# A delta-rule attention with two expert layers on one core: solves placed earlier, expert blocks six steps behind attention

## What is computed

```
k_n = k / (norm(k) + 1e-6);  state = 0            # 48 x 48 per head
for t in range(768):
    y[t]  = q[t] @ state
    v_old = k_n[t] @ state
    state = state + beta[t] * outer(k_n[t], v[t] - v_old)
```

```
P = exp(x @ w_gate - max);  8 times: rows, then columns of P normalised, P *= N / E
out = sum over e of P[:, e] * (relu(x @ w1[e]) @ w2[e])
```

## Time and profile before

| | us |
|---|---|
| median of 3 runs | 2405.42 (2396.09 to 2406.7) |
| the profiled execution | 2400.81 |
| its span, first to last instruction | 2399.0 |
| TensorE busy | 2252.4 (94%) |
| DVE busy | 1015.1 (42%) |
| ScalarE busy | 611.0 (25%) |
| GpSimd busy | 106.1 (4%) |
| mean granted clock of TensorE | 0.958 |
| a kT load (512 KB), issue to landing, median | 5.2 |

### The profile page before, as it was taken

How to read it: one execution, slowest core, us unless ns; L and a number is a source line. 1 busy time by engine, 2 the same in 40 slices (tenths; PEclk the granted TensorE clock), 3 DMA queues, 4 the chain that set the end, 5 groups by cost and what they waited for, 6 DMA issues and landing times.

```text
span 2399.0 us, 43062 instructions
## 1 busy us (share of the span) xinstructions
PE 2252.4 (94%) x18100; PEld 2089.4 (87%) x18100; DVE 1015.1 (42%) x1831; ACT 611.0 (25%) x1021; POOL 106.1 (4%) x106
## 2 busy tenths in 40 slices
PE   3878988898999999999999999999999996899998
PEld 3878988798999999899899899989999886899998
DVE  6655554426432323333233333333333325566664
ACT  2322222231111111111111111111111122566664
POOL 0000000000000000000000000000000000222221
PEclk7789989899999999999999999999999997899999
DMA  7554344322000000000000000000000012666651
GB/s 246 171 146 120 114 122 115 102 76 100 27 27 1 27 1 27 27 1 27 1 27 27 1 27 1 27 26 2 1 1 1 14 40 79 221 228 209 232 199 61
DMA packets 153378, 173.92 MB, mean 72 GB/s; under 512 B 82124, under 2 KB 113008, under 8 KB 153218
## 3 DMA queue, kind: packets, MB, share of 16 engines
q1 hardware_dynamic: 148354, 159.29, 20.8%
q0 software_dynamic: 4864, 12.20, 1.4%
HBM read 145.50 MB, written 28.71 MB: 73 GB/s over the span
## 4 chain that ended last, share of the span: by engine, by line
PE 88%; DVE 5%; DMA 2%; SPq 2%; issue 2%; ACT 1%; POOL 0%; POOLq 0%; ACTq 0%; DVEq 0%
PE psA L1480 21%; PE psH L1495 15%; PE psB L1480 8%; PE psB L1495 7%; PE psY L1495 7%; PE psY L1589 7%; PE psA L1265 4%; PE psH L1381 4%; PE psA L1576 3%; PE psB L1576 3%; PE psY L1396 3%; PE psB L1364 1%; PE psB L1354 1%; PE psB L1323 1%; DMA r_scratch<-sr 1%
## 5 line engine op out<-in xcount | busy, mean ns | idle before, releaser
L1480 PE MATMUL psA<-X,wh 128*128 128x512 f32 x1440 | 455.0, 397 | 5.5 <-DVE wl L1081 4.1
L1088 DVE SCALAR_TENSOR_TENSOR hl<-psA,hh 128x512 fp32r<-128x512 f32 x240 | 165.8, 691 | 647.7 <-ACT hh L760 647.6
L760 ACT ACTIVATE hh<-psA 128x512 fp32r<-128x512 f32 x240 | 143.3, 597 | 854.7 <-PE psA L1480 854.7
L1480 PEld LDWEIGHTS psA<-X,wh 128*128 128x128 f32 x1440 | 269.6, 190 | 52.4 <-issue 7.1
L1480 PE MATMUL psA<-X,wl 128*128 128x512 f32 x720 | 288.7, 401 | 0.0
L1495 PE MATMUL psH<-wh,hh 128*128 128x384 f32 x672 | 228.4, 340 | 0.0
L1495 PE MATMUL psH<-wh,hl 128*128 128x384 f32 x672 | 227.2, 338 | 0.0
L1495 PE MATMUL psH<-wl,hh 128*128 128x384 f32 x672 | 225.8, 336 | 0.0
L1088 DVE SCALAR_TENSOR_TENSOR hl<-psB,hh 128x512 fp32r<-128x512 f32 x96 | 66.4, 691 | 277.7 <-ACT hh L760 277.7
L1480 PE MATMUL psB<-X,wh 128*128 128x512 f32 x576 | 179.2, 392 | 0.0
L1212 DVE TENSOR_TENSOR vl<-vs,vh 128x768 fp32r<-128x768 f32 x152 | 145.1, 957 | 58.1 <-ACT vh L797 56.6
(11 more groups left out here) (235 smaller groups left out, 4243.4 us busy)
## 6 DMA issues: line engine op xcount, KB each, us to landing
vs<-v_d SPq DMA_DIRECT2D x38, 768.0 KB, 6.2
vs<-v_d SPq DMA_DIRECT2D x19, 1536.0 KB, 12.1
ws<-w_d SPq DMA_DIRECT2D x28, 768.0 KB, 6.1
kT<-kT_d SPq DMA_DIRECT2D x17, 512.0 KB, 5.2
qT<-qT_d SPq DMA_DIRECT2D x15, 512.0 KB, 4.2
a_scratch<-an SPq DMA_DIRECT2D x12, 512.0 KB, 3.5
kq<-kn_d SPq DMA_DIRECT2D x6, 768.0 KB, 6.4
vn<-vn_d SPq DMA_DIRECT2D x12, 384.0 KB, 4.2
```

Source lines behind the costliest of these rows:

```text
L760: act.activation(hh[kk % 3][:, :], ps_h[kk % (2 if last else 3)], ACT.Relu).then_inc(hh_ready, 1)
L1088: dve.scalar_tensor_tensor(hl[b][:, :], ps_h[bank], 0.0, hh[b][:, :].bitcast(F32), ALU.max, ALU.subtract).then_inc(hl_ready, 1)
L1480: mm = pe.matmul(to, a[half][:, c, col], X[:, 2 * g:2 * g + 2, b, c, :], start=(n == 0), stop=(n == 3 * KC - 1))
```

## The change

`LAG` goes from 8 to 6: each block stands two steps earlier. The parts of chunks 2 to 11 too stand two steps earlier; those of chunks 0 and 1 stay, so blocks 0 and 1 come beside chunk 1's outputs. Solves 2 to 5 end at step 16n - 9 where they ended at 16n - 4, with `cross` now at 16n - 3; solve 1 ends at step 8 (was 12, with `cross` at 13, was 15). Solve 2 has its 31 rows in 11 steps. The blocks for solves 3 to 5 are loaded at steps 24, 40, 56. Products, weight splits, key norms of the start move up by one or two steps. The inverse of pair 0 is loaded by ScalarE, and `kP[2]`, `qP[0]` are issued ahead of `store_inverse(0)`. Chunks 4 and 5 use the A buffer 2 instead of 3; waits follow that.

The core of the diff:

```diff
-LAG = 8
+LAG = 6
-AT_KS = [None, 4] + [13 + KF * (c - 2) for c in range(2, NC)]
+AT_KS = [None, 4] + [11 + KF * (c - 2) for c in range(2, NC)]
...
-SOLVE_SECOND = [4, 3, 3, 3, 2, 2, 2, 2, 2, 2, 2, 2, 2]
-AT_SOLVED = [None] + [16 * n - 4 for n in range(1, NG)]
+SOLVE_SECOND = [4, 4, 4, 4, 3, 3, 3, 3, 3]
+SOLVE_THIRD = [2, 3, 3, 3, 3, 3, 3, 3, 3, 3, 2]
+AT_SOLVED = [None, 8] + [16 * n - 9 for n in range(2, NG)]
...
-AT_MIX = [None] * EARLY + [3, 4, 5, 6] + [AT_KS[c - 4] + 4 for c in range(8, NC)]
-AT_GRAM = [None] * EARLY + [8, 10] + [AT_KS[c - 4] + 2 for c in range(6, NC)]
-AT_PART = [None] * 3 + [12, 13, 14]
-AT_SPLIT = {4: (0, 0), 5: (0, 1), 7: (1, 0), 8: (1, 1)}
+AT_MIX = [None] * EARLY + [1, 2, 4, 5] + [AT_KS[c - 4] + 4 for c in range(8, NC)]
+AT_GRAM = [None] * EARLY + [8, 9, AT_KS[2] + 3] + [AT_KS[c - 4] + 2 for c in range(7, NC)]
+AT_PART = [None] * 3 + [11, 12, 13]
+AT_SPLIT = {2: (0, 0), 3: (0, 1), 5: (1, 0), 6: (1, 1)}
...
-            return c % NA if c < EARLY else NA
+            return c % NA if c < EARLY else 2 if c < 6 else NA
...
-                store_inverse(0)
-                store_a(3)
-                for c in range(2):
-                    load_inverse(c)
-                load_blocks(1)
                 load_pair(kP[2], kT, 2, s_kP[2])
                 sp.wait_ge(m_done, 2)
                 load_pair(qP[0], qT, 2, s_qP[0])
+                store_inverse(0)
+                store_a(3)
+                load_blocks(1)
                 load_first(1)
...
-                    if s >= 12 and s % 16 == 12 and s // 16 + 2 < NG:
+                    if s == 12:
+                        load_blocks(2)
+                    if s in range(24, 16 * NG - 24, 16):
                         load_blocks(s // 16 + 2)
...
                     if n >= 1:
-                        act.wait_ge(an_out[NA], 16 * min(2 * n, NC - EARLY))
+                        act.wait_ge(inv_out, 32 * n)
+                    if n >= 2:
+                        act.wait_ge(an_out[NA], 16 * min(2 * n - 2, NC - 6))
...
                 transpose_blocks(0)
+                for c in range(2):
+                    load_inverse(act, c)
...
-                            act.wait_ge(an_out[2], 16)
+                            act.wait_ge(an_out[2], 48)
...
-                    if s == AT_SPLIT_END - 1:
+                    if s == AT_SPLIT_END - 2:
                         reduce_part(2)
```

More of the change, by code:

```diff
@@ L86, in solve_plan @@
     for n in range(2, NG):
+        steps = SOLVE_THIRD if n == 2 else SOLVE_STEPS
         done = 0
-        for i, k in enumerate(SOLVE_STEPS):
-            plan[AT_SOLVED[n] - len(SOLVE_STEPS) + 1 + i] = (n, done, done + k)
+        for i, k in enumerate(steps):
+            plan[AT_SOLVED[n] - len(steps) + 1 + i] = (n, done, done + k)
             done += k
@@ L309, in a_buffer @@
         def a_buffer(c):
-            return c % NA if c < EARLY else NA
+            return c % NA if c < EARLY else 2 if c < 6 else NA
         def a_stored(c):
-            return 16 * (c // NA + 1 if c < EARLY else c - EARLY + 1)
+            return 16 * (c // NA + 1 if c < EARLY else c - 2 if c < 6 else c - 5)
         def mix_bank(c):
@@ L344, in unit_after, with load_inverse @@
             return u - 1 if f == 0 and 1 <= u <= NC else None
+        def load_inverse(engine, c):
+            n, par = c // 2, c % 2
+            engine.wait_ge(inv_out, 32 * (n + 1))
+            if c >= 2:
+                engine.wait_ge(o_done, c - 1)
+                engine.wait_ge(w_done, c - 1)
+            else:
+                engine.wait_ge(s_zero, 3)
+            for k in range(2):
+                for g in range(2):
+                    p0 = g * C + k * BS
+                    q0 = ((par * 2 + g) * 2 + k) * NJ
+                    engine.dma_start(rs[par][p0:p0 + BS, :, k * BS:(k + 1) * BS],
+                                     r_dram[n, q0:q0 + NJ, :, :].rearrange("j t s -> t j s")).then_inc(s_inv[par], 16)
+                    if k == 0:
+                        engine.dma_start(ts[par][p0:p0 + BS, :, :],
+                                         t_dram[n, q0:q0 + NJ, :, :].rearrange("j t s -> t j s")).then_inc(s_inv[par], 16)
         with nc.Block() as block:
@@ L391, in load_corner @@
                         sp.dma_start(aos[par][p0:p0 + BS, :, :], a_dram[c, p0:p0 + BS, :, 0:BS]).then_inc(s_ao[par], 16)
[L393 to L409, removed]
                 def load_first(half):
@@ L484, in _ @@
                         for par in range(2):
-                            load_inverse(2 * AT_SOLVED.index(s - 2) + par)
+                            load_inverse(sp, 2 * AT_SOLVED.index(s - 2) + par)
                     if s - 2 in AT_X[0:NC - 2]:
@@ L632, in split_first @@
                     act.wait_ge(w0_in[half], 32)
+                    if half == 1 and layer == 1:
+                        act.wait_ge(s_red, 3)
                     to, src = (wh1, fh1) if layer == 0 else (wh2, fh2)
@@ L911, in scale @@
                         dve.wait_ge(an_out[0], 16)
-                    if c >= EARLY:
+                    elif c in (4, 5):
+                        dve.wait_ge(an_out[2], 16 * (c - 3))
+                    elif c >= 6:
                         dve.wait_ge(inv_out, 32 * (c // 2 - 1))
-                        if c > EARLY:
+                        if c > 6:
                             dve.wait_ge(an_out[NA], a_stored(c - 1))
@@ L954, in unit_out @@
                         else:
-                            dve.wait_ge(an_out[2], 16)
+                            dve.wait_ge(an_out[2], 48)
                     dve.tensor_copy(to, ps_u[1]).then_inc(y0b_ready, 1)
```

## The result

The changed kernel takes 2383.57 us (median of 5 runs, 2378.84 to 2386.1) against 2405.42 (5 runs, 2396.09 to 2406.7): ratio 0.9912, 95% interval 0.989 to 0.9934. It is 0.9% faster, where 2.2% was forecast; 2383.6 lies above the range of 2336 to 2374. The profiled execution has a span of 2384.2 us against 2399.0.

The account below looks back on a forecast made before the run. TensorE was taken as the bound, with idle holes from waits for the inverse and slow clock after them. Savings of 42.6 us steady and 8 at the start, 50.6, set at 52, gave 2352 us; 8-in-10 range 2336 to 2374.

Parts of the forecast that it names:

- The wait goes, margin 7.8 us: Steady part: with the transpose earlier, the inverse arrives 7.8 us before TensorE reaches the even chunk's `cross`, ending that wait.
- So the slow clock adds 2.9 us ... sum over four: 12 us: Steady part: low TensorE clock behind four waits for the inverse costs 12 us together, saved when the waits go.
- 42.6 us: Steady part's total saving: 32.6 us of waits plus 12 of slow clock, less 2 for DVE.
- The even chunk's key load stands behind that store and waits with it ... Nothing.: Steady part, SP's queue: key load lands at 209, wanted at 212.34; no cost, bounds 0 to 2 us a pair.
- I take off 2 us (0 to 10): Steady part: late y0 copies and DVE's solve rows beside the even chunk's heavy steps cost 2 us.
- 8 us saved: Start, to the first unit's end: the first `give` behind the y0 copy comes 8 us earlier, bounds 0 to 21.
- No row shows a DMA issued by ScalarE ... bounds 0 to 3 us later ... I take 0, as it is the same work.: Start: ScalarE issuing the first inverse's 12 loads takes 6.3 us, as on SP, so adds 0 us.
- Loads of the inverse until 127 to 129 ... four block loads 2.2 us ... 136 to 138.: Start, SP's queue behind Gram 5: inverse loads, then block loads, so solve 2's blocks land at 136 to 138 us.
- 2.6 us of new wait ahead of Gram 5: Start: Gram of chunk 5, a step earlier, waits about 2.6 us for DVE's scaling of chunk 4's.
- 0 for the megabyte moved: Start: kP[2] and qP[0], 1 MB, moved ahead of the first inverse's store on SP, cost 0 us.
- rival 2: New DVE or inverse-load waits take half: steady gain 20 us, total 28; 2377 us (2366 to 2390), chance 0.16.
- Rival 3: Slower: transpose stays late, even chunk's keys wait behind it in SP's queue, 15 us lost; 2412 us, chance 0.04.

Follow-up runs that it names:

- e9: e8 with the odd half of every pair's inverse loaded behind the next key load instead of ahead of it; 2357.11 us, ratio 0.9799 to the kernel before.
- e2: Changed kernel with the next qT and kT loads ahead of the block loads and inverse store in SP's step; 2377.11 us, ratio 0.9904 to before.
- e1: Changed kernel with the first pair's 12 inverse loads back on SP, ahead of solve 1's block loads; 2376.75 us, ratio 0.9898 to before.
- e3: Changed kernel, ScalarE still issuing, with SP's large loads held until the first pair's inverse has landed; 2376.12 us, one run.
- e10: Kernel before with only kP[2] and qP[0] (1 MB) issued ahead of the first inverse's store; 2398.61 us, one run.
- e4: Changed kernel with solve 2's rows laid out otherwise: one in steps 19 and 20, four in steps 21 to 23; 2383.05 us, one run.
- e7: Changed kernel with the edits of e1 and e2 together; 2369.21 us, ratio 0.9859 to the kernel before.
- e11: e8 with the three 768 KB key loads issued behind chunk 2's inverse loads; 2365.23 us, one run.
- e6: Kernel before, LAG 8, with only solves 2 to 5 ending six steps ahead of use and q, k loads ahead of the store; 2371.18 us, ratio 0.9847.
- e8: e7 with e4's step table and chunk 3's inverse loads behind solve 2's block loads and Gram 6's key load; 2366.18 us, ratio 0.9841 to before.

## Why the prediction was wrong

**"The wait goes, margin 7.8 us"** was right. No `cross` from chunk 4 on waits for the inverse, and `sr` starts behind the odd chunk's `ww` copy. **"So the slow clock adds 2.9 us ... sum over four: 12 us"** was right in size: with the waits gone for good, in e9, busy time falls by 12.4 us. That it fits so well is in part luck: half of 9.4 and of 7 us is 4.7 and 3.5, where the sum took 4 and 2.6, so that by halves it would have been 14.6. **42.6 us** for the steady part was there to be had: 44.0 in e9, with orders of SP's queue that the sum did not price. The changed kernel itself got 26.5, because of two steps:

- **"The even chunk's key load stands behind that store and waits with it ... Nothing."** The list was one short. The qT load stands in the same place, for `outputs` of the odd chunk, and is wanted at 292.8 in the trace of after, where it left SP at 291.68. Two waits of 4.6 and 4.0 us came of it, each with a short stretch at low clock behind. Taking this load out of the way (e2) gave 8.8 us between the marks. It uncovered a wait of 3.5 us for keys in the same queue; e9, which has none left there, is another 8.6 us shorter, in part by DVE's table and by a clock that fell less often.
- **"I take off 2 us (0 to 10)"** for DVE. The steady wait for `pm` is 3.2 us, for y0 1.4 (6.4 less 5.0 at the start). With some slow clock this lies inside the bounds.

By the two windows, 16 us are missing: holes gave 22.2 us where I had 30.6 (32.6 - 2), and low clock 4.4 where I had 12. The two kinds of new wait, 8.6 + 3.2 = 11.8 us against the 2 taken off, less 2.3 us by which the y0 waits shrank, account for nearly all of the missing holes. Behind each of them the clock is low for a while; in e2, where the waits for qT are gone, busy time is 4.3 us less. That the rest of the 7.6 us comes of these stretches too is argued.

**"8 us saved" at the start** failed by 17 us, in two separate steps:

- **"No row shows a DMA issued by ScalarE ... bounds 0 to 3 us later ... I take 0, as it is the same work."** This was the larger error. The issues took 14.6 us, not 6.3, of which the last two 7.05. I priced the number of issues, from SP's row where the engines had only these loads to serve. The number that mattered is what else fills the engines while the issuing engine still has something to hand over, and what that engine computes next: ScalarE was on the path to `cross`'s second half, SP was not. Together with the `cross` that I had 1.5 us later (0 to 3) and that came 4.4 later, this edit costs 8 to 13.5 us of span (three pairs of profiles; 6.8 by the medians of e1). With ScalarE issuing and the block loads beside it, the first `cross` is at 63.7 to 65.1 in five profiles, without at 59.6 to 61.4 in eight. The Trainium skill ("DMA: Bandwidth & Descriptors", "Issuing engines are not separate DMA queues") says that DMAs issued by different engines run on the same 16 DMA engines and interleave. The later `cross` agrees with that; the prediction gave such sharing 1.5 us, or 2 to 3 were it even, and e3, with the large loads held, shows 3.9.
- **"Loads of the inverse until 127 to 129 ... four block loads 2.2 us ... 136 to 138."** Even with SP issuing (e1) no gain is left. The key loads go out at 118.3 and not 114.3, the inverse's loads last until 134.6, and the block loads until 140.7. I had counted four of the eight block loads (5.4 us), and Gram 5 came 4 us later than I had it. The wait for chunk 2's inverse did shrink, from 10.8 to 1.7, as forecast (about 2), and turned into one of 7.3 (7.8 in e1) for the keys of Gram 6: the load that stands behind the block loads, which the sum had left out of the queue.

Right were 2.6 us of new wait ahead of Gram 5 (2.42), the y0 wait and the slow stretch still there, and 0 for the megabyte moved (e10). From the handover to the end I had 1839; it is 1838.7.

**Rivals.** The time fell into the region of rival 2 (2377, 2366 to 2390, chance 0.16), but not by its mechanism as a whole: DVE beside heavy steps made 3.2 us, the other new waits of the steady part came from a load queued behind a store that waits, and the start was lost as told above. The rival's second half, "the inverse behind SP's block loads", named the right queue and the wrong load. Rival 3 had the mechanism (keys behind the store) and put it at 0.04, since I asked there only whether it could turn the sign, and not what a small lateness would cost. It remains open how the 4.4 us of the first `cross` divide between the block loads' bytes, the number of their pieces and ScalarE as the issuer; no run separated them.

## What to carry to other kernels

When a wait on one queue is removed by moving work earlier, write down every entry that stands behind the moved step in that queue, with the time at which each is wanted, not only those that the edit touches. An engine that computes on the critical path should not issue transfers while others fill the DMA engines: price its issues by what else is moving. And where large transfers lead a queue of small ones, the order decides only who waits, so put last what is wanted last; splitting the inverse's loads by chunk, with e4's table, went with 2369 to 2357 us (e7 to e9; ratios 0.9859 and 0.9799) without removing a byte, though the profiles show only a part of that as waits for loads.

## What the runs showed of the hardware

- An engine's last DMA issues can be far longer than its first. The same pair took 1.02 us on SP with only small loads moving, 1.67 on ScalarE with the large loads held, 7.05 and 7.30 with them in flight. In e11 eight block loads took 13.46 us behind 2.3 MB of keys; behind no large load they took 5.2 to 5.5 (before, e1, e3).
- The mean busy share of the 16 DMA engines can stand above 1. From 60 to 64 us it was 0.80 at 124 GB/s before the change, and 1.61 at 125 GB/s after, in the stretch where two engines' small loads shared them (1.57 at 127 GB/s in e3, with the large loads held). Twice the packet time, the same bytes: the share alone says nothing of speed there.

```profile
60.00:64.00 4.00, 2.00 (x66) 1.89 (x68) 0.00 (x0) 1.17 (x2) 0.00 (x0) 0.50 0.80 124
```
```profile
60.00:64.00 4.00, 0.00 (x0) 0.00 (x0) 0.00 (x0) 0.00 (x0) 0.00 (x0) 0.50 1.61 125
```

- In e6 a gap of 2.0 us was followed by a granted clock of 0.50 (1.2 GHz) for some 12 us, where one of 0.9 us in the same code of before left it at 1.00. The length of the gap alone does not decide: waits of 1.36 and 1.62 us in e8 were followed by 0.50 for some 3 and 6.5 us, and one of 1.49 us in e7 left the clock at 1.00. One profile's start was 6 us later with it, and the runs of one kernel spread over 14 to 21 us; that the gap is the cause of the whole spread is argued, not shown (e6: 2361.7 to 2375.8; before: 2393.8 to 2414.5).
